# Thresholded attention: scores stay in three PSUM slots, GpSimd splits k and normalises

## The reference, cut to what matters

```python
scores = matmul(q, k.T) / sqrt(64)
thresh = max(scores, axis=-1) - tau          # tau = 0.02
scores = where(scores >= thresh, scores, -1e9)
attn = exp(scores - max(scores)); attn = attn / (sum(attn) + 1e-9)
out = matmul(attn, v)                        # (8, 8, 576, 64)
```

## Time and profile before

| | |
|---|---|
| Median of 3 runs | 1396.44 us (1392.83 to 1396.92) |
| Profiled execution | its span is 1394.9 us from first to last instruction; no other time of it is given |
| Attention | the first 663 us |
| Mixing | the remaining 732 us |
| Granted TensorE clock | 0.993 of full speed over the span |

### The profile page before, as it was taken

One profiled execution on the slowest core, in us unless ns is written; L12 is line 12 of the kernel. 1 busy time (PEld: TensorE's weight loads), 2 busy tenths in 40 slices (PEclk: granted clock), 3 DMA queues, 4 the chain that ended last, 5 costly groups with the idle time before them and its releaser, 6 DMA issues.

```text
span 1394.9 us, 30382 instructions
## 1 busy us (share of the span) xinstructions
PE 1351.6 (97%) x9632; PEld 1147.0 (82%) x9632; DVE 1023.9 (73%) x2507; ACT 870.9 (62%) x2058; POOL 148.4 (11%) x151
## 2 busy tenths in 40 slices
PE   5899999999999999997899999999999999999998
PEld 4677777777777677774899999999999999999997
DVE  3789998999999998986776665666565666756544
ACT  4788888888888888885654445444553445544532
POOL 1212122212212122210200000000000000000000
PEclk9999999999999999999899999999999999999999
DMA  6533333333333333322201110011101110011000
GB/s 196 159 92 95 105 108 100 91 105 105 104 96 91 107 106 100 91 79 80 65 1 33 33 33 17 27 33 33 33 6 38 33 33 17 17 41 33 16 8 31
DMA packets 141079, 90.46 MB, mean 65 GB/s; under 512 B 96192, under 2 KB 125120, under 8 KB 140992
## 3 DMA queue, kind: packets, MB, share of 16 engines
q1 hardware_dynamic: 138368, 83.06, 21.1%
q10 hardware_dynamic: 2624, 6.29, 1.3%
HBM read 70.29 MB, written 25.31 MB: 69 GB/s over the span
## 4 chain that ended last, share of the span: by engine, by line
PE 51%; DVE 1%; ACT 0%; issue 0%; DVEq 0%
PE kv_ps L815 15%; PE kv_ps L896 15%; PE vr_ps L815 14%; PE y_ps L880 7%; DVE xm_lo L1014 0%; DVE mixed L1008 0%; ACT mixed L928 0%; DVE x L1067 0%; ACT xm_hi L936 0%; ACT y L945 0%; DVE g_lo L1040 0%; DVE x_lo L1072 0%; DVE square L1025 0%; DVE gated L1035 0%; ACT x_hi L992 0%
## 5 line engine op out<-in xcount | busy, mean ns | idle before, releaser
L549 DVE SCALAR_TENSOR_TENSOR probs<-neg_scores,threshold,probs 128x576 f32<-128x576 f32 x288 | 256.6, 891 | 14.5 <-ACT threshold L477 11.9
L542 DVE TENSOR_SCALAR_CACHE_REDUCE neg_scores<-score_ps 128x576 f32<-128x576 f32 x288 | 214.2, 752 | 36.7 <-PE score_ps L395 28.1
L475 ACT ACTIVATE probs<-neg_scores,neg_max 128x576 f32<-128x576 f32 x288 | 223.4, 776 | 3.6 <-DVE neg_scores L542 3.0
L350 PEld LDWEIGHTS block_ps<-ident,probs 128*128 128x128 f32 x1280 | 138.9, 141 | 91.6 <-issue 63.0
L458 ACT ACTIVATE probsT<-block_ps 128x512 f32<-128x512 f32 x291 | 168.1, 596 | 70.9 <-PE block_ps L350 69.6
L350 PE MATMUL block_ps<-ident,probs 128*128 128x128 f32 x1280 | 204.3, 282 | 1.6 <-DVE k_lo L571 0.5
L446 PE MATMUL out_ps<-probsT,v_nat 128*64 128x320 f32 (+1 forms) x1024 | 167.0, 427 | 3.5 <-DVE x_out L586 3.0
L395 PE MATMUL score_ps<-k_lo,qT 128*128 128x288 f32 x512 | 167.3, 342 | 1.2 <-DVE k_lo L571 1.2
L815 PE MATMUL kv_ps<-xm_hi,w_lo 128*128 128x288 f32 x512 | 152.6, 298 | 15.5 <-DVE xm_lo L1014 12.2
L815 PE MATMUL kv_ps<-xm_hi,w_hi 128*128 128x288 f32 x512 | 152.6, 298 | 0.0
L815 PE MATMUL kv_ps<-xm_lo,w_hi 128*128 128x288 f32 x512 | 152.4, 298 | 0.0
(11 more groups left out here) (94 smaller groups left out, 3054.1 us busy)
## 6 DMA issues: line engine op xcount, KB each, us to landing
k_nat<-in_k SPq DMA_DIRECT2D x128, 128.0 KB, 2.5
recip_rows<-recip_scratch SPq DMA_DIRECT2D x64, 144.0 KB, 2.9
x_scratch<-x_out SPq DMA_DIRECT2D x32, 288.0 KB, 2.2
out<-y SPq DMA_DIRECT2D x36, 256.0 KB, 2.0
q_nat<-in_q SPq DMA_DIRECT2D x32, 256.0 KB, 2.7
v_nat<-in_v SPq DMA_DIRECT2D x32, 256.0 KB, 2.6
w_stage<-packed SPq DMA_DIRECT2D x32, 192.0 KB, 2.5
x_in<-x_scratch SPq DMA_DIRECT2D x8, 578.0 KB, 4.0
```

The source lines that it names most:

```text
L350: return nc.tensor.transpose(out, in_, ident[:])
L475: nc.scalar.activation(tile(i), neg_scores[:, (cc + i) % 2, :], ACT.Exp, bias=neg_max[:, i:i + 1], scale=-1.0).then_inc(exp_done, 1)
L542: nc.vector.tensor_scalar(neg_scores[:, (cc + i) % 2, :].rearrange("p (a b) -> p a b", a=2), score_ps[(cc + i) % 2][:, :, 0:HALF], -1.0, F ...
L549: nc.vector.scalar_tensor_tensor(tile(i), neg_scores[:, (cc + i) % 2, :], threshold[:, i:i + 1], tile(i), ALU.is_le, ALU.mult, accum_out=r ...
```

## The change: what it does

- The scores stay in PSUM, in three slots of two banks (tile i in slot i % 3). `copy` becomes `max`, a reduction that writes only the negated row maximum. `exp` and `mask` read PSUM. A slot is free again when its `mask` is done.
- The other two banks (`aux_ps`) take every transposition and, in turn with them, the results of `pv`. The ten visits of `pv` become two, of twenty matmul instructions each, and ACT copies each result to SBUF (`x_raw`).
- ACT copies the transposed k unsplit (`k_raw`); POOL splits it (`split_k`), one half for each head, with 64 more columns beside the second.
- POOL adds 1e-9 to the row sums (`sums`) and multiplies output by reciprocals (`normalize`) in DVE's place.
- The three lists are reordered. SP loads the weight slice before the reciprocals' trip.

The core of the diff:

```diff
 PE_PLAN = steps("""
-    scores0 probs6- scores1 probs7- pv0- pv1- pv2- q0 scores2 pv3- probs8- scores3 pv4-
-    probs0 k0 scores4 rem1- scores5 pv5- probs1 k1 pv6- probs2 pv7- scores6 q1 pv8- rem0
-    scores7 probs3 kq0 scores8 pv9- probs4 probs5
+    scores0 probs3- probs7- scores1 pv0- scores2 probs6- probs8- scores3 q0 rem1- scores4
+    probs0 pv1- kq0 scores5 k0 rem0 scores6 probs2 k1 scores7 probs1 q1 scores8 probs4 probs5
 """)
 ACT_PLAN = steps("""
+    probs3- exp8- probs7- exp0 exp1 pv0- probs6- probs8- q0 rem1- probs0 exp2 exp3 exp4 pv1-
+    kq0 k0 rem0 exp5 probs2 k1 exp6 probs1 q1 exp7 probs4 probs5
 """)
 DVE_PLAN = steps("""
+    max8- max0 max1 mask8- recip0- mask0 mask1 max2 max4 max3 mask2 mask3 max5 mask4 max6
+    mask5 max7 mask6 mask7
 """)
...
# SP, for run c
+                def run(it, c):
+                    if c <= PAIRS - 3:
+                        sp.wait_ge(aux_full, turns(it, prepared(c - 1)))
                         load_qk(it, c + 2)
+                    if c > 0:
+                        ...
+                            sp.wait_ge(w_split, count(it, c, 2, -2))
+                        load_w(it, c - 1)
+                        spread(it, c - 1)
...
+                        store_x(it, c - 1)
...
# POOL
+                def split_k(it, c, run):
+                    for h in range(2):
+                        ready = max(number(run, ("k", h, False)), number(run, ("kq", 0, False)))
+                        wait(aux_copied, turns(it, ready + 1))
+                        ...
+                        nc.gpsimd.tensor_copy(hi[:, to], k_raw[:, to]).then_inc(k_steps, 1)
+                        wait(k_steps, count(it, c, 4, 2 * h + 1))
+                        ...
+                        nc.gpsimd.tensor_tensor(lo[:, to], k_raw[:, to], hi[:, to].bitcast(F32),
+                                                ALU.subtract).then_inc(k_steps, 1)
+                def sums(it, c):
+                    wait(probs_ready, count(it, c, TILES, TILES))
+                    nc.gpsimd.tensor_scalar_add(row_sum[:, c % 2, :], ..., 1e-9).then_inc(sum_ready, 1)
+                def normalize(it, c):
+                    wait(aux_copied, turns(it, number_of(c, "pv", 1) + 1))
+                    wait(rows_loaded, count(it, c, 32, 32))
+                    ...
+                    nc.gpsimd.tensor_tensor(x_out[:, 0:MAIN].rearrange("p (q t) -> p t q", t=FULL),
+                        x_raw[:, 0:MAIN].rearrange(...), recip_rows[:, 0:MAIN].rearrange(...), ALU.mult)
+                    nc.gpsimd.tensor_tensor(x_out[:, MAIN:S], ...).then_inc(x_ready, 1)
+                def run(it, c):
+                    if c < PAIRS - 1:
+                        wait(aux_full, turns(it, prepared(c - 1)))
+                        split_q(it, c + 1)
+                    if c > 0:
+                        sums(it, c - 1)
+                        normalize(it, c - 1)
+                    if c < PAIRS - 1:
+                        split_k(it, c + 1, c)
+                    if c > 0:
+                        split_w(it, c - 1)
...
# PE, scores
+                            if i == 0:
+                                pe.wait_ge(aux_copied, turns(it, prepared(c - 1)))
+                                pe.wait_ge(k_steps, count(it, c, 4, 2))
+                            if i == 1:
+                                pe.wait_ge(k_steps, count(it, c, 4, 4))
+                            if c > 0 or i >= SLOTS:
+                                pe.wait_ge(probs_ready, count(it, c, TILES, i + 1 - SLOTS))
...
# DVE
-                            nc.vector.tensor_scalar(neg_scores..., score_ps..., -1.0, FLT_MAX, ALU.mult, ALU.min,
-                                accum_out=neg_max[:, i:i + 1]).then_inc(scores_copied, 1)
+                            nc.vector.tensor_reduce(neg_max[:, i:i + 1], scored(i), mybir.AxisListType.XY, ALU.max,
+                                                    negate=True).then_inc(max_ready, 1)
...
                             nc.vector.scalar_tensor_tensor(
-                                tile(i), neg_scores[:, (cc + i) % 2, :], threshold[:, i:i + 1], tile(i),
-                                ALU.is_le, ALU.mult,
+                                tile_halves(i), scored(i), threshold[:, i:i + 1], tile_halves(i),
+                                ALU.is_ge, ALU.mult,
                                 accum_out=row_sum[:, cc % 2, i:i + 1]).then_inc(probs_ready, 1)
                         elif kind == "recip":
-                            nc.vector.tensor_scalar_add(row_sum..., 1e-9).then_inc(sum_ready, 1)
                             dve.wait_ge(sum_ready, count(it, cc, 1, 1))
                             nc.vector.reciprocal(recip[:], row_sum[:, cc % 2, :]).then_inc(recip_ready, 1)
```

More of the change, by code:

```diff
@@ L65 @@
 assert PER_PAIR % 2 == 0
[L68 to L70 removed]
 def first(plan):
[L75 removed]
+    return [x for x in plan if not x[2]]
 def last(plan):
@@ L85, in drain, with numbered, ranked @@
     return [x for x in plan if x[2]]
[L89 to L93, removed]
+def numbered(plan):
+    return {step: n for n, step in enumerate(x for x in plan if x[0] in GROUPS)}
+def ranked(plan, kind):
+    order = [i for k, i, before in plan if k == kind and not before]
+    order += [i for k, i, before in plan if k == kind and before]
+    return {i: n for n, i in enumerate(order)}
+MAX_TURN = ranked(DVE_PLAN, "max")
+MASK_TURN = ranked(DVE_PLAN, "mask")
+EXP_TURN = ranked(ACT_PLAN, "exp")
+assert list(MASK_TURN) == list(EXP_TURN) == sorted(MASK_TURN)
 def attention(nc, q, k, v, tau, small_loads, x_first, weight_copies, wraw, x_scratch, recip_scratch, w_hi, w_lo, wcols):
@@ L183, in count_loaded, with number, number_of, turns @@
             return it * (16 * loads) + 16 * loads * (c // 2 + 1)
[L185 to L196, removed]
+        def number(run, step):
+            if run < 0:
+                return numbered(FIRST_PREPARE)[step]
+            if run == 0:
+                return PREPARED + FIRST_RUN[step]
+            start = PREPARED + len(FIRST_RUN) + (run - 1) * PER_PAIR
+            if run < PAIRS - 1:
+                return start + FULL_RUN[step]
+            if run == PAIRS - 1:
+                return start + LAST_RUN[step]
+            return start - PER_PAIR + len(LAST_RUN) + DRAIN_RUN[step]
+        def number_of(c, kind, i):
+            before = (kind, i, True) in FULL_RUN
+            return number(c + before, (kind, i, before))
+        def turns(it, n):
+            return it * (2 * PER_PAIR) + n
+        def prepared(run):
+            return 1 + max(number(run, x) for x in FIRST_PREPARE)
         def walk(run, eng, plan):
-            run(FIRST_PREPARE, 0, -1, numbered(FIRST_PREPARE, PER_PAIR), {})
-            run(first(plan), 0, 0, NUMBERS, {})
+            run(FIRST_PREPARE, 0, -1)
+            run(first(plan), 0, 0)
             with eng.Fori(0, (PAIRS - 2) // 2) as it:
[L203 to L206, removed]
+                run(plan, it, 1)
+                run(plan, it, 2)
+            run(last(plan), 0, PAIRS - 1)
+            run(drain(plan), 0, PAIRS)
         with nc.Block() as block:
@@ L362, in run @@
                         if kind in GROUPS:
[L363 to L371, removed]
+                            g = number(c, (kind, i, before))
+                            if g >= 2:
+                                pe.wait_ge(aux_copied, turns(it, g - 1))
+                            bank = aux_ps[g % 2]
+                            blocks = bank[:].rearrange("p (t q) -> p t q", t=4)
+                        if kind == "scores":
                             par = c % 2
                             if i == 0:
[L376 to L382, removed]
+                                pe.wait_ge(aux_copied, turns(it, prepared(c - 1)))
[4 more added lines that the diff above has]
+                                pe.wait_ge(probs_ready, count(it, c, TILES, i + 1 - SLOTS))
                             for half in range(2):
@@ L426, in run @@
+                            pe.wait_ge(q_steps, count(it, c + 1, 2, 2))
+                            transpose(blocks[:, 0, :], q_split[:, MIX, :, :])
+                            last = transpose(blocks[:, 1, :], k_nat[:, (c + 1) % 2, MIX, :, :])
                         elif kind == "pv":
-                            second, t = divmod(i, FULL + 1)
-                            if t == 0:
-                                done = group(numbers, earlier, "probs", MIX if second else FULL - 1, before)
-                                wait_copied(pe, it, c, done)
-                                wait_copied(pe, it, c, done - 1)
@@ L530, in run @@
+                def run(plan, it, c):
                     for kind, i, before in plan:
                         cc = c - 1 if before else c
-                        if kind in GROUPS:
-                            g = numbers[kind, i, before]
-                            bank = block_ps[g % 2]
-                            done = blocks_copied[g % 2]
```

(4 more changed lines are left out.)

272 lines of the change are left out of this document (117 added, 155 removed).

## The result

| | median | runs |
|---|---|---|
| Before | 1395.1 us | 1392.83 to 1396.92, 4 runs |
| After | 1422.8 us | 1420.39 to 1423.96, 4 runs |

The ratio is 1.0196, 95% interval 1.0179 to 1.0213: slower by 27.7 us. The forecast was 1440 us, its range 1400 to 1472.

A forecast was written before the change was run, and what follows sets the result against it. PE's queue was taken to bound the kernel before, POOL's loop after: 20.97 us a pair against 19.53, 30 rounds of 1.45 us, 43.5 us, plus about 1 at the end, giving 1440 us, range 1400 to 1472.

The forecast's parts named there:

- What the change takes away: Attention, per pair: PE's work put at 18.1 us, DVE relieved of 4.4 us, ACT at 16.9 us.
- the two banks: PE's four groups in a row on two PSUM banks, waiting for ACT: some 0.7 us a pair.
- the first rival: Loop shorter or not closed; PE and ACT order decides, 18.8 us a pair, 1374 us; chance 0.12.
- the loop: Waits from one `split_k` end to the next, once a pair: 20.97 us, above today's 19.53.
- The chain through POOL: POOL's strict list makes `split_k` wait behind `normalize` for the reciprocals; nine items sum to 20.97 us a pair.
- the trip: Reciprocals' store to DRAM and load back until used, in front of `normalize`: put at 6.15 us.
- my bound: Range for strided `normalize` on POOL: 1.6 us up to 2.8 us if writes double; 1.9 taken.
- item 7: The reciprocals' trip through DRAM, 6.15 us, with SP assumed free because its loads are out 5 us earlier.
- Start and end: Before and after the paired rounds: start left at nothing, end about 1 us more for `normalize` on POOL.
- Contention: POOL and DVE sharing SBUF: `mask` reading PSUM takes no lock, so both engines run at their shortest rows.
- The second: Rival: the loop is just hidden, 19.4 to 19.7 us a pair, 1394 to 1401 us; chance 0.05.
- The third and fourth: Rivals: POOL still collides with DVE, 1507 us, chance 0.06; POOL's operations otherwise longer, 1470 to 1500 us, chance 0.07.

The follow-up runs named there:

- the grouped `pv`: Kernel before the change with only PE's list altered, the ten `pv` visits in two groups of five: 1437.2 us (ratio 1.0302).
- The kernel in which PE is full: Changed kernel with `split_k` in front of `normalize` on POOL and `sums` back on DVE: 1366.8 us (ratio 0.9807).
- the operation behind the trip or in front of it: Changed kernel plus a superfluous 576-column POOL subtraction for 30 pairs: behind `normalize` 1457.8 us, in front of it 1417.1 us.
- the two single edits: Changed kernel with only `sums` back on DVE: 1402.3 us; with only `split_k` in front of `normalize` on POOL: 1397.8 us.
- the two combinations: Changed kernel with `sums` on DVE and `split_k` in front of `normalize`: 1366.8 us; the same plus a superfluous subtraction inside `split_k`: 1378.3 us.
- once POOL's order was mended: Changed kernel with `split_k` before `normalize` and `sums` on DVE: 1366.8 us; with only POOL reordered (`sums`, `split_q`, `split_k`, `normalize`, `split_w`): 1369.3 us.

## Why the prediction was right

**What bounds the kernel before.** PE's queue, as far as the runs go: PE is busy throughout, and DVE's work could be cut by 0.8 us a pair without any gain (1395.5 us). But the queue is not free to be reordered; the grouped `pv` shows that the other engines' lists are woven to it.

**What the change takes away.** PE's work was put at 18.1 us a pair, with 0.7 more for the two banks in the first rival. The kernel in which PE is full paces at 18.77. The sum fits; its parts fit only roughly. PE in that kernel (timeline, `probs6- probs8-` first, then the place with four groups in a row):

```profile
417.49 1.04 PE L389 MATMUL aux_ps<-ident,probs 128*128 128x128 f32 x8
418.28 0.38 PE L428 MATMUL score_ps<-k_lo,qT 128*128 128x288 f32 x1
...
430.60 0.38 PE L428 MATMUL score_ps<-k_lo,qT 128*128 128x288 f32 x1
...
431.44 1.22 PE L389 MATMUL aux_ps<-ident,probs 128*128 128x128 f32 x8
432.41 0.38 PE L428 MATMUL score_ps<-k_lo,qT 128*128 128x288 f32 x1
```

From start to start, `probs3- probs7-` takes 0.97 us where `probs6- probs8-` takes 0.79, and `scores0` in front of them 0.84 where `scores3` takes 0.61: the two banks cost some 0.4 us there, not 0.7, and the rest is score tiles, groups and `pv` that are a little longer than I put them. The pace is 0.76 us a pair better than before, 24 us, and in the changed kernel the loop hides that; how much of it is the grouped `pv` no run shows. `max` costs 0.753 us on average, inside 0.65 to 0.8. DVE's work fell from 17.8 to 13.6 us a pair (busy time of the stretch times the pace), 4.2 where 4.4 were forecast; the one part of it that was tried alone, L555, was worth nothing.

**The chain through POOL.** Right as a mechanism: the operation behind the trip or in front of it (35 us or none), the two single edits and the two combinations all moved as the loop says, and not as the rivals named beside them. Its sum was 0.42 us a round too high in the round shown. Three items are off by more than 0.15 us: `normalize` measured 1.50 us, not 1.9, so this strided output cost nothing that shows and the bottom of my bound, 1.6, was the better value; `split_k` 4.82, not 5.2, where I had given gaps between instructions that overlap; the trip 6.74 (mean 6.59), not 6.15, because I took the row of the last pair. The last trip of the kernel after is 6.28 us too (681.14 to 687.42), so other pairs' work beside it is the likely cause; it wasn't tried.

**The size.** It is less good than the total looks. The forecast gave the loop 43.5 us, 30 rounds of 1.45. The 29 intervals between the first and the last grew by 0.79 us each, 22.9 in all, about half: the loop was 20.38 us and not 20.97, which is 17 us, and the rest is that I set a full round against the average of 19.53, where the same intervals before took 19.59, and counted one round more. Part of that came back by luck, through terms that the forecast had at nothing: 6.0 us in the first interval, where SP was not free as item 7 assumes (its store was 8.6 us late, see above), and 3.5 us in the last one, which no run explains. Without these 9.5 us the result would be near 1413, still inside the range.

**Start and end.** I left the start at nothing; it gave back 4.0 us, 44.5 to 40.5 at the first reciprocal. The likely reason is that the first run no longer fills groups of the missing pair with dummy transposes; that wasn't tried. Behind the last reciprocal the end cost 0.2 us, not 1.

**Contention.** `mask` reads PSUM now and doesn't vary any more, and the POOL operations stay at their shortest rows of before (1.62 us, and 1.40 to 1.75). The kernel after, durations in ns min/median/max:

```profile
L555 DVE SCALAR_TENSOR_TENSOR probs<-score_ps,threshold,probs x288: 764/817/820, 20.2 to 676.9; 128x576 f32<-128x576 f32 x144
...
L335 POOL TENSOR_TENSOR k_lo<-k_raw,k_hi x64: 1397/1406/1434, 14.1 to 657.0; 128x576 fp32r<-128x576 f32 x64
```

The lock rule of the Trainium skill, "SBUF — State Buffer", section "SBUF: two separate sides", fits both: two SBUF inputs took it, one from PSUM doesn't.

**The rivals.** The first (an order of PE and ACT decides, 1374 us) is what came once POOL's order was mended: 1367 and 1369. The second (the loop just hidden, 19.4 to 19.7) did not come: 20.57, and 20.38 without the first and the last interval. The third and fourth (collisions, longer POOL operations) did not occur.

## What to carry to other kernels

When work moves to an engine that is mostly idle, don't ask whether it has the time, but what stands in front of each result in its list: here 10 us of idle time a pair and a superfluous operation of 1.4 us showed that place, and not load, decides. Follow every wait once round until you are back at its start, and put the operation that waits longest (a trip through DRAM) behind those that others wait for. Look at the first round by itself too: loads needed once, much later, stood in front of the first trip. A new order of one engine, like the grouped `pv`, can need new lists on the others: alone it cost 43 us.

## What the runs showed of the hardware

- POOL's 512-column multiplication with an output stride took 1.30 us, in line with plain ones of 384 and 576 columns at 1.01 and 1.41; on DVE, 256 such columns took 0.63 where 512 plain ones took 0.69.
- A subtraction whose two inputs are the same tile took 1.14 us on POOL for 576 columns against 1.41 for two different ones.
- The trip of 4.6 KB through DRAM and back took from 6.1 to 7.2 us from pair to pair in one and the same execution. The store up to the issue of the load back took 2.35 to 2.43 us, the load back up to its use 3.7 to 4.8.
